# Who turns the output: TensorE or VectorE, in a fused convolution, gated layer and squared layer

## The chip, the core and the metric

The kernel runs on one core of a Trainium2 chip. The metric is the device time of one execution in microseconds (us), as the median of the runs shown. Times in the trace are counted from the first instruction of the profiled execution.

## What is computed

Softmax-weighted causal convolution over 7 tokens (8 heads of 24 channels, 4 batches of 4096 tokens, 192 channels), then a gated layer (192 to 1536 to 192) and a squared-ReLU layer (192 to 2048 to 192), all in fp32:

```python
x_unf = x_pad[:, idx, :].reshape(B, S, K, H, group)
x = np.einsum('hk,bskhg->bshg', softmax(weight), x_unf).reshape(B * S, D)
x = (1 / (1 + np.exp(-(x @ w_gate)))) * (x @ w_val) @ w_out1
h = np.maximum(x @ w_in2, 0.0)
return (h * h) @ w_out2
```

## The kernel before

The 4096 tokens of a batch are cut into 32 blocks of 128; a block holds those 128 tokens of all four batches, so each tile of the hidden layers is 128 features by 512 columns. Channels lie on the partitions throughout. Input tokens are turned into that layout by VectorE in squares of 32 (`transpose_x`, L805: 32 instructions for one block, 16 of 32x128 elements and 16 of 32x64), and the output is turned back at the end.

Each fp32 value is held as a high part (`hi`, a cast by ScalarE) and a low part (`lo`, a subtraction by VectorE), and three products of the parts are summed. Because 192 channels are 128 plus 64, TensorE works in pairs of matmuls, one on the lower 64 partitions and one on the upper 64, that run side by side.

A block goes through two stages. The **gated** stage has T1 = 12 steps. In step t TensorE computes `in1(t)`, 9 pairs (L400, L401) into one of two pairs of PSUM banks of `hp`; ScalarE takes the sigmoid of one bank (L625); VectorE multiplies it by the other bank (`hidden`, L767), which signals `prod_done`; ScalarE casts the product to `hi` (`round_hi`, L611) and VectorE subtracts to get `lo` (`rest_lo`, L781), which signals `lo1_done`. TensorE runs `out1(t - 3)`, 5 pairs (L466 to L472), after `in1(t)`, and after the last step it runs `out1(8)` and `out1(9)` in a row. The **squared** stage has 16 tiles, two per `in2(p)`: ReLU by ScalarE (L628), the square by VectorE (L771), then `hi` and `lo` as above, and `out2` two pairs of tiles behind.

`in1(t)` may begin when the product of tile t - 2 has been read out of its banks (`prod_done`, L435). `out1(t)` begins when `lo` of tile t is there (L486). On VectorE the product of tile t stands ahead of the `lo` of tile t - 1.

The steady loop runs 29 times. One pass is `squared(i - 1)` and then `gated(i + 1)`, so in a gated stage the finished output z of block i - 1 waits to be evacuated, turned and stored:

- step 2: ScalarE copies half of the accumulator (`z_copy`) and VectorE adds (`z_add`, L860) into `z` and `z_parts`;
- SyncE (SP) moves the two halves of `z_parts` that belong to the other partitions (`cross_z`, L290, L291), GpSimd (POOL) adds them (`add_z_rest`, L375), which signals `z_rest_done`;
- TensorE turns the output (`turn`, L493 to L517) after step TR1 = 5: six pairs of transposes into the free banks of `hp`. To have a free pair there, `pair1` flips the parity of the banks from step 6 on;
- ScalarE copies the four pieces to `o_sb` (`turn_copy`, L678, L683), SP stores them (`store`, L295).

Beside that, VectorE in the same gated stage turns the input of the next block (steps 0 to 7, four squares in each), runs its first four convolution taps (EARLY = 4, steps 8 to 11; L812 is the first tap, L815 the others, two instructions each), and at step 8 makes the low part of the second layer's input (`x1_low`, L798). At step 8 ScalarE casts that input (`x1_round`, L659, L661), and GpSimd then computes its remaining low part (`low_of_x1_rest`, L368). The other three taps run in the squared stage (steps 1, 3, 6). SP's order in one pass of the loop is `load_x`, `cross_y1`, `spread_x0`, `cross_z`, `store`, `spread_x1`; `spread_x1` brings the second layer's input to the other partitions and `in2(0)` waits for it.

Outside the loop there are a first gated stage, a second without any output to turn, one light squared and one light gated stage at the end (nothing left to load), and the last squared stage, in which the output of block 30 is turned. The last block's output is turned after all other work.

Of the kernel before, what the change touches and what calls it, by code (L numbers as in the profile page):

```python
# [11 lines left out]
P = 128  # L12
R = 64
# [5 lines left out]
TR1, TR2 = 5, 3  # L19


def conv_gated_squared_mlp(nc, x, weight, w_gate, w_val, w_out1, w_in2, w_out2, out):
# [14 lines left out]
    EARLY = 4  # L37
# [6 lines left out]
    with ExitStack() as ctx:  # L44
# [63 lines left out]


# [31 lines left out]
        sig_w_done = sem("sig_w_done")  # L141
        w_hi = sem("w_hi")
# [16 lines left out]
        sq_done = sem("sq_done")  # L159
# [5 lines left out]
        z_added = sem("z_added")  # L165

# [53 lines left out]

        def pair1(t, prev):

            return (t + (1 if prev and prev[0] == 2 and t > TR1 else 0)) % 2

        def pair2(p, prev):
            return (p + (1 if prev[0] == 2 and p > TR2 else 0)) % 2
# [13 lines left out]
        def _(sp):  # L240
# [47 lines left out]
            def cross_z(j):  # L288
                sp.wait_ge(z_added, 2 * j + (1 if isinstance(j, int) and j == NB - 1 else 2))
                sp.dma_start(z_moved[lower, :, :], z_blocks[upper, :, 0, :]).then_inc(z_crossed, 16)  # L290
                sp.dma_start(z_moved[upper, :, :], z_blocks[lower, :, 1, :]).then_inc(z_crossed, 16)  # L291
# [28 lines left out]
            cross_z(NB - 3)  # L320
            store(NB - 3)
            spread_x1(NB - 2)
# [9 lines left out]
        def _(pool):  # L332
# [38 lines left out]
            def add_z_rest(j):  # L371
                pool.wait_ge(z_crossed, 32 * (j + 1))
                for half, of in enumerate((lower, upper)):
                    v = z_blocks[of, :, half, :]
                    nc.gpsimd.tensor_tensor(v, v, z_moved[of, :, :], ALU.add) \  # L375
                        .then_inc(z_rest_done, 1)
# [17 lines left out]
        def _(pe):  # L394
# [28 lines left out]
            def in1(j, t, prev):  # L423
                turns = prev and prev[0] == 2
# [3 lines left out]
                if t < 2 and turns:  # L428
                    pe.wait_ge(relu_done, T2 * prev[1] + T2 - 2 + 2 * t)
                elif turns and t == TR1 + 1:  # L430
                    pe.wait_ge(prod_done, T1 * j + t)
                elif turns and t == TR1 + 2:
                    pe.wait_ge(turn_copied, 4 * prev[1] + 4)
# [4 lines left out]
                low, up = into(pair1(t, prev), w1, x0_home(j), columns(t))  # L438
                low.then_inc(gate_ready, 1)
                up.then_inc(val_ready, 1)  # L440

            def in2(j, p, prev):
                if p == 0:
                    pe.wait_ge(x1_spread, 48 * j + 48)
                turns = prev[0] == 2
                if p < 2 and not turns:
                    if p == 0:
                        pe.wait_ge(prod_done, T1 * prev[1] + T1)
                elif turns and p == TR2 + 1:
                    pe.wait_ge(relu_done, T2 * j + 2 * p)  # L450
                elif turns and p == TR2 + 2:
                    pe.wait_ge(turn_copied, 4 * prev[1] + 4)
                else:
                    pe.wait_ge(relu_done, T2 * j + 2 * p - 2)
                low, up = into(pair2(p, prev), w2, x1_home(j), columns(p))
                low.then_inc(hid_ready, 1)
                up.then_inc(hid_ready, 1)
# [35 lines left out]
            def turn(j, free):  # L493


                last = isinstance(j, int) and j == NB - 1
                a, b = hp[:, 0, :], hp[:, 1, :]
                pe.wait_ge(*free)
                if last:
                    pe.wait_ge(z_added, 2 * j + 2)  # L500
                else:
                    pe.wait_ge(z_rest_done, 2 * j + 2)
# [5 lines left out]
                if last:  # L508
                    mm.then_inc(turned, 1)
                    a, b = hp[:, 2, :], hp[:, 3, :]  # L510
                    pe.wait_ge(z_rest_done, 2 * j + 2)
                    pe.sem_inc(turn_begun, 1)
# [4 lines left out]
                mm.then_inc(turned, 1 if last else 2)  # L517
# [23 lines left out]
            def gated(j, prev):  # L541
                rest_ = trailing(prev)
                for t in range(T1):
                    if prev is None and t < 2:
                        if t == 0:
                            first_tiles()
                    else:
                        in1(j, t, prev)
                    some_of(rest_)
                    if t >= LAG1:  # L550
                        out1(j, t - LAG1, prev)
                    if prev and prev[0] == 2 and t == TR1:
                        turn(prev[1], (prod_done, T1 * j + t))
                out1(j, T1 - LAG1, prev)

            def squared(j, prev):
# [3 lines left out]
                for p in range(T2P):  # L560
# [5 lines left out]
                    if prev[0] == 2 and p == TR2:  # L566
                        turn(prev[1], (relu_done, T2 * j + 2 * p))
# [21 lines left out]
            turn(NB - 1, (relu_done, T2 * NB))  # L589

        @block.scalar
        def _(act):
# [14 lines left out]
            def round_hi(kind, j, t, prev):  # L607
# [4 lines left out]
                else:  # L612
                    act.wait_ge(sq_done, T2 * j + t + 1)
                    act.copy(hi[:, t % RING, :], hid_t[:, t % 4, :]).then_inc(hi2_done, 1)  # L614

            def activate(kind, j, t, prev):
                if t >= 2 or (prev and prev[0] == kind):
                    s, n = (prod_done, T1) if kind == 1 else (sq_done, T2)
                    act.wait_ge(s, n * j + t - 1)
                elif prev:  # L620
                    s, n = (prod_done, T1) if prev[0] == 1 else (sq_done, T2)
                    act.wait_ge(s, n * prev[1] + n - 1 + t)
                if kind == 1:
                    act.wait_ge(gate_ready, T1 * j + t + 1)
                    act.activation(act_t[:, t % 2, :], hp[:, 2 * pair1(t, prev), :], ACT.Sigmoid).then_inc(sig_done, 1)  # L625
                else:
                    act.wait_ge(hid_ready, T2 * j + t + 1)
                    act.activation(act_t[:, t % 2, :], hp[:, 2 * pair2(t // 2, prev) + t % 2, :], ACT.Relu) \  # L628
# [44 lines left out]
            def turn_copy(j):  # L673
                last = isinstance(j, int) and j == NB - 1
                act.wait_ge(o_room, 16 * (j + 1))
                act.wait_ge(turned, 2 * j + (1 if last else 2))
# [3 lines left out]
                if last:  # L680
                    act.wait_ge(turned, 2 * j + 2)
                for half in range(2):
                    act.copy(o_sb[:, half:B:2, P:D], hp[:, (2 if last else 0) + half, B * R:G * R].rearrange(  # L683
# [12 lines left out]
            def gated(j, prev, pieces_at={}):  # L696
                for t in range(T1):
# [4 lines left out]
                    if t == TR1 + 1 and prev and prev[0] == 2:  # L702
                        turn_copy(prev[1])
# [11 lines left out]
            def squared(j, prev, load_next=True):  # L715
                for t in range(T2):
# [4 lines left out]
                    if t == 2 * TR2 + 2 and prev[0] == 2:  # L721
                        turn_copy(prev[1])
# [5 lines left out]
                    activate(2, j, t, prev)  # L728
                    if t:
# [26 lines left out]
        def _(dve):  # L756
            def hidden(kind, j, t, prev):
# [6 lines left out]
                if kind == 1:  # L764
                    dve.wait_ge(sig_done, T1 * j + t + 1)
                    dve.wait_ge(val_ready, T1 * j + t + 1)
                    dve.tensor_tensor(hid_t[:, t % 4, :], hp[:, 2 * pair1(t, prev) + 1, :], act_t[:, t % 2, :],  # L767
                                      ALU.mult).then_inc(prod_done, 1)
                else:
                    dve.wait_ge(relu_done, T2 * j + t + 1)  # L770
                    dve.tensor_tensor(hid_t[:, t % 4, :], act_t[:, t % 2, :], act_t[:, t % 2, :],  # L771
                                      ALU.mult).then_inc(sq_done, 1)
# [70 lines left out]
            def y1_add(j):  # L843
# [3 lines left out]
                if not (isinstance(j, int) and j < 2):  # L847
                    dve.wait_ge(z_rest_done, 2 * j - 2)
                dve.tensor_tensor(y1_parts[:], acc[:, 1, :], acc_up[:, 1, :], ALU.add).then_inc(y1_added, 1)

            def z_add(j):
                last = isinstance(j, int) and j == NB - 1
                if not (isinstance(j, int) and j == 0):
                    dve.wait_ge(turned, 2 * j)
# [7 lines left out]
            def add_last_z_rest():  # L862
                dve.wait_ge(z_crossed, 32 * NB)
# [4 lines left out]
            def last_of(prev):  # L868
                rest_lo(prev[0], prev[1], (T1 if prev[0] == 1 else T2) - 1)

# [6 lines left out]
            def gated(j, prev, load_next=True):  # L877
                for t in range(T1):
# [24 lines left out]
            def squared(j, prev, load_next=True):  # L903
                for t in range(T2):
# [4 lines left out]
                    if load_next and t in (1, 3, 6):  # L909
                        conv_tap(j + 2, EARLY + t // 2 - t // 6)  # L910
                    if load_next and t == 6:
# [7 lines left out]
                    hidden(2, j, t, prev)  # L919
# [62 lines left out]
```

## Time and profile before

| what | value |
|---|---|
| median of 3 runs | 2385.01 us (2384.59 to 2385.89) |
| profiled execution, its own time | 2385.3 us |
| profiled execution, its span | 2383.1 us |
| TensorE matmul busy | 2351.4 us, 99% |
| TensorE weight load busy | 2119.0 us, 89% |
| VectorE busy | 1824.3 us, 77% |
| ScalarE busy | 1162.3 us, 49% |
| GpSimd busy | 181.9 us, 8% |
| granted TensorE clock | 0.998 of full speed |

The busy time of an instruction in the trace runs from its start to its end; instructions of one engine overlap at their ends, so a duration is longer than the distance to the next start. Where an engine is full, it is the distance between starts that counts. Idle time of an engine is listed with what it waited for. A share over the whole span says nothing of a single stage: VectorE's 77% is a mean over gated and squared stages.

### The profile page before, as it was taken

What the parts mean: (1) busy time and instruction counts of PE and PEld (TensorE: products, weight loads), DVE (VectorE), ACT (ScalarE), POOL (GpSimd) and SP (SyncE); (2) the same over time, 40 slices, a digit from 0 to 9 for tenths busy, and PEclk for the clock granted to TensorE, in tenths of its full rate; (3) what the DMA queues carried; (4) which work ended last, traced back from release to release, by engine and by line L of the source; (5) the groups of instructions that cost most, each with busy time, mean ns of one, the idle gap of its engine ahead of it and who ended that gap; (6) DMA issues with size and microseconds to landing.
All of it is one profiled execution on the core that took longest, in us unless ns stands there. A gap on an engine that the chain in (4) does not pass through costs nothing.

```text
span 2383.1 us, 54234 instructions
## 1 busy us (share of the span) xinstructions
PE 2351.4 (99%) x20880; PEld 2119.0 (89%) x20880; DVE 1824.3 (77%) x3468; ACT 1162.3 (49%) x2208; POOL 181.9 (8%) x164
## 2 busy tenths in 40 slices
PE   6999999999999999999999999999999999999998
PEld 5898998889899989998998888899989888998987
DVE  6777787777787877877777878778777787787755
ACT  3545454454544454544455444455445454454544
POOL 3300000000010000000000000001000000000110
PEclk9999999999999999999999999999999999999999
DMA  5211111111111111111111111111111111111110
GB/s 133 61 48 29 40 48 31 46 29 42 46 38 39 43 28 46 48 31 46 29 42 46 31 46 32 38 46 48 31 46 29 40 48 31 46 29 42 41 39 19
DMA packets 99901, 99.39 MB, mean 42 GB/s; under 512 B 8736, under 2 KB 86048, under 8 KB 99872
## 3 DMA queue, kind: packets, MB, share of 16 engines
q1 hardware_dynamic: 99856, 98.99, 16.9%
q8 instruction: 20, 0.33, 0.1%
q14 instruction: 9, 0.07, 0.0%
q10 hardware_dynamic: 16, 0.00, 0.0%
HBM read 19.27 MB, written 12.58 MB: 13 GB/s over the span
## 4 chain that ended last, share of the span: by engine, by line
PE 98%; DVE 1%; ACT 0%; issue 0%; DMA 0%; POOL 0%; SPq 0%; ACTq 0%; DVEq 0%
PE hp L400 36%; PE hp L401 18%; PE acc L466 17%; PE acc L471 11%; PE acc L467 9%; PE acc L472 6%; DVE y L815 1%; DMA stage<-in_moe_w_val_dram 0%; PE hp L506 0%; PE hp L507 0%; PE hp L515 0%; DVE hid_t L767 0%; POOL wo L358 0%; DMA moved<-z_parts 0%; SPq L263 0%
## 5 line engine op out<-in xcount | busy, mean ns | idle before, releaser
L400 PE MATMUL hp<-xs,w 64*128 64x512 f32 x5760 | 1407.1, 388 | 13.3 <-DVE hid_t L767 5.5
L401 PE MATMUL hp<-xs,w 64*128 64x512 f32 x5760 | 1406.9, 388 | 0.0
L400 PEld LDWEIGHTS hp<-xs,w 64*128 64x128 f32 x5760 | 1060.0, 185 | 121.5 <-DVE hid_t L767 7.4
L401 PEld LDWEIGHTS hp<-xs,w 64*128 64x128 f32 x5760 | 1060.0, 185 | 23.6
L781 DVE TENSOR_TENSOR lo<-hid_t,hi 128x512 fp32r<-128x512 f32 x896 | 617.1, 689 | 7.8
L625 ACT ACTIVATE act_t<-hp 128x512 f32<-128x512 f32 x384 | 230.0, 599 | 674.0 <-PE hp L400 674.0
L771 DVE TENSOR_TENSOR hid_t<-act_t 128x512 f32<-128x512 f32 x512 | 381.6, 746 | 228.4 <-ACT act_t L628 228.1
L466 PE MATMUL acc<-hi,wo 64*128 64x512 f32 x1792 | 549.5, 386 | 0.0
L467 PE MATMUL acc<-hi,wo 64*128 64x512 f32 x1792 | 549.4, 386 | 0.0
L767 DVE TENSOR_TENSOR hid_t<-hp,act_t 128x512 f32<-128x512 f32 x384 | 265.1, 690 | 246.1 <-ACT act_t L625 237.8
L628 ACT ACTIVATE act_t<-hp 128x512 f32<-128x512 f32 x512 | 302.7, 598 | 297.4 <-PE hp L401 180.0
L614 ACT CAST hi<-hid_t 128x512 fp32r<-128x512 f32 x512 | 316.5, 618 | 148.2 <-DVE hid_t L771 142.0
L466 PEld LDWEIGHTS acc<-hi,wo 64*128 64x128 f32 x1792 | 330.0, 184 | 31.4
L472 PE MATMUL acc<-lo,wo 64*128 64x512 f32 x896 | 346.1, 386 | 0.0
L471 PE MATMUL acc<-lo,wo 64*128 64x512 f32 x896 | 346.1, 386 | 0.0
L466 PE MATMUL acc<-lo,wo 64*128 64x512 f32 x896 | 346.1, 386 | 0.0
L467 PE MATMUL acc<-lo,wo 64*128 64x512 f32 x896 | 346.1, 386 | 0.0
L471 PE MATMUL acc<-hi,wo 64*128 64x512 f32 x896 | 346.1, 386 | 0.0
L472 PE MATMUL acc<-hi,wo 64*128 64x512 f32 x896 | 346.1, 386 | 0.0
L467 PEld LDWEIGHTS acc<-hi,wo 64*128 64x128 f32 x1792 | 330.0, 184 | 7.4
L805 DVE STREAM_TRANSPOSE xT<-xin 32x128 f32<-32x128 f32 x960 | 258.0, 269 | 28.2
L611 ACT CAST hi<-hid_t 128x512 fp32r<-128x512 f32 x384 | 235.4, 613 | 11.3 <-DVE hid_t L767 11.3
(69 smaller groups left out, 1897.8 us busy)
## 6 DMA issues: line engine op xcount, KB each, us to landing
xs<-xs SPq DMA_DIRECT2D x160, 256.0 KB, 3.8
xs<-y_rest SPq DMA_DIRECT2D x128, 128.0 KB, 3.1
out_dram<-stage SPq DMA_DIRECT2D x32, 384.0 KB, 2.6
xin<-in_x_dram SPq DMA_DIRECT2D x30, 384.0 KB, 4.2
moved<-y_parts SPq DMA_DIRECT2D x32, 128.0 KB, 2.2
moved<-z_parts SPq DMA_DIRECT2D x64, 64.0 KB, 2.0
stage<-in_moe_w_out_dram SPq DMA_DIRECT2D x7, 384.0 KB, 5.0
stage<-in_moe_w_in_dram SPq DMA_DIRECT2D x12, 128.0 KB, 3.0
```

Of the source, the lines that this page charges most:

```text
L400: low = pe.matmul(hp[:, 2 * pair, :], w[lower, wk, c], xs[lower, xk, :], start=s, stop=e)
L401: up = pe.matmul(hp[:, 2 * pair + 1, :], w[upper, wk, c], xs[upper, xk, :], start=s, stop=e)
L466: pe.matmul(acc[:, 0, :], w[lower], v[lower], start=s, stop=e)
L467: pe.matmul(acc[:, 2, :], w[upper], v[upper], start=s, stop=e)
L471: pe.matmul(acc[:, 1, :], rest_w[lower], v[lower], start=s, stop=e)
L472: mm = pe.matmul(acc[:, 3, :], rest_w[upper], v[upper], start=s, stop=e)
L614: act.copy(hi[:, t % RING, :], hid_t[:, t % 4, :]).then_inc(hi2_done, 1)
L628: act.activation(act_t[:, t % 2, :], hp[:, 2 * pair2(t // 2, prev) + t % 2, :], ACT.Relu) \
L767: dve.tensor_tensor(hid_t[:, t % 4, :], hp[:, 2 * pair1(t, prev) + 1, :], act_t[:, t % 2, :], ALU.mult).then_inc(prod_done, 1)
L771: dve.tensor_tensor(hid_t[:, t % 4, :], act_t[:, t % 2, :], act_t[:, t % 2, :], ALU.mult).then_inc(sq_done, 1)
L781: dve.tensor_tensor(lo[:, t % RING, :], hid_t[:, t % 4, :], hi[:, t % RING, :].bitcast(F32), ALU.subtract).then_inc(done, 1)
L805: dve.transpose(dst, src).then_inc(xT_ready, 1)
```

## The change

1. The turn of the output leaves TensorE for all blocks but the last. VectorE turns it (`turn_z`) in 24 squares of 32x128 straight from `z` and `z_parts` to `o_sb`, three per step in steps 4 to 11 of a gated stage (two per step in steps 4 to 15 of the last squared stage). The flip of banks in `pair1` and `pair2` and the waits around the turn are gone, and so are ScalarE's four copies.
2. In the squared stage ScalarE squares the odd tiles (`square_odd`), VectorE only the even ones.
3. EARLY is 3 instead of 4: the input's squares are spread over steps 0 to 8 and the first tap stands at step 9; four taps fall in the squared stage (steps 1, 3, 5, 7).
4. SP's order in the loop is `cross_z`, `spread_x1`, `store` instead of `cross_z`, `store`, `spread_x1`. The store waits for the 24 squares.
5. `cross_z` moves the upper half of `z_parts` to the lower in one transfer, and GpSimd adds it in one 64x512 instruction instead of two of 64x256.
6. `in2(0)` waits for the product of tile 10 instead of tile 11, since the banks no longer flip.

```diff
-    EARLY = 4
+    EARLY = 3
...
+        for c in range(D // Q):
+            of, ch = (z, slice(c * Q, (c + 1) * Q)) if c < P // Q else (z_parts, slice(c * Q - P, (c + 1) * Q - P))
+            for m in range(P // Q):
+                tok = slice(m * Q, (m + 1) * Q)
+                o_squares.append((of[ch, :].rearrange("c (b s) -> c b s", b=B)[:, :, tok],
+                                  o_sb[tok, :, c * Q:(c + 1) * Q]))
...
             def store(j):
-                sp.wait_ge(turn_copied, 4 * j + 4)
+                if isinstance(j, int) and j == NB - 1:
+                    sp.wait_ge(turn_copied, 4)
+                else:
+                    sp.wait_ge(o_turned, O_SQUARES * (j + 1))
...
                 cross_z(i - 1)
+                spread_x1(i)
                 store(i - 1)
-                spread_x1(i)
...
-                if p < 2 and not turns:
-                    if p == 0:
-                        pe.wait_ge(prod_done, T1 * prev[1] + T1)
...
+                if p < 2 and prev[0] == 1:
+                    pe.wait_ge(prod_done, T1 * prev[1] + T1 - 1 + p)
...
-                    if prev and prev[0] == 2 and t == TR1:
-                        turn(prev[1], (prod_done, T1 * j + t))
...
+            def square_odd(j, t, prev):
...
+                act.wait_ge(relu_done, T2 * j + t + 1)
+                act.activation(hid_t[:, t % 4, :], act_t[:, t % 2, :], ACT.Square).then_inc(odd_sq_done, 1)
...
+            def turn_z(j, part, parts):
+                if part == 0:
+                    dve.wait_ge(o_room, 16 * (j + 1))
+                    dve.wait_ge(z_added, 2 * j + 1)
+                for n in range(part * O_SQUARES // parts, (part + 1) * O_SQUARES // parts):
+                    if n == REST_SQUARES:
+                        dve.wait_ge(z_rest_done, j + 1)
+                    src, dst = o_squares[n]
+                    dve.transpose(dst, src).then_inc(o_turned, 1)
...
+                    if t >= 4 and prev and prev[0] == 2:
+                        turn_z(prev[1], t - 4, T1 - 4)
...
-                    hidden(2, j, t, prev)
+                    if t >= 4 and prev[0] == 2:
+                        turn_z(prev[1], t - 4, T2 - 4)
+                    if t % 2 == 0:
+                        hidden(2, j, t, prev)
```

VectorE's program, from the end of step 6 to the product of step 8 of a gated stage in the loop, before (`xT<-xin` turns the input, `hid_t` is the product, `lo` the low part, `xs<-y,xs` is `x1_low`):

```order
L781 TENSOR_TENSOR lo<-hid_t,hi 128x512
L805 STREAM_TRANSPOSE xT<-xin 32x2x32 x4
L765 REGISTER_ALU
L767 TENSOR_TENSOR hid_t<-hp,act_t 128x512
L781 TENSOR_TENSOR lo<-hid_t,hi 128x512
L834 REGISTER_ALU
L835 REGISTER_ALU
L812 TENSOR_SCALAR y<-xT,taps 128x512
L812 TENSOR_SCALAR y<-xT,taps 128x256
L798 TENSOR_TENSOR xs<-y,xs 128x512
L765 REGISTER_ALU
L767 TENSOR_TENSOR hid_t<-hp,act_t 128x512
```

The same stretch after (`stage<-z` turns the output; `o_sb` lies in the tile `stage`):

```order
L785 TENSOR_TENSOR lo<-hid_t,hi 128x512
L809 STREAM_TRANSPOSE xT<-xin 32x4x32 x4
L883 STREAM_TRANSPOSE stage<-z 32x4x32 x3
L769 REGISTER_ALU
L771 TENSOR_TENSOR hid_t<-hp,act_t 128x512
L785 TENSOR_TENSOR lo<-hid_t,hi 128x512
L809 STREAM_TRANSPOSE xT<-xin 32x2x32 x4
L883 STREAM_TRANSPOSE stage<-z 32x4x32 x3
L802 TENSOR_TENSOR xs<-y,xs 128x512
L769 REGISTER_ALU
L771 TENSOR_TENSOR hid_t<-hp,act_t 128x512
```

Ahead of each product there now stand seven transposes where there were four, the input's last squares have moved into step 8, and the first tap (L812) has moved to step 9.

VectorE in steps 10 and 11 of the same stage, before:

```order
L815 SCALAR_TENSOR_TENSOR y<-xT,taps,y 128x512
L814 REGISTER_ALU
L815 SCALAR_TENSOR_TENSOR y<-xT,taps,y 128x256
L765 REGISTER_ALU
L767 TENSOR_TENSOR hid_t<-hp,act_t 128x512
L781 TENSOR_TENSOR lo<-hid_t,hi 128x512
```

and after:

```order
L819 SCALAR_TENSOR_TENSOR y<-xT,taps,y 128x512
L818 REGISTER_ALU
L819 SCALAR_TENSOR_TENSOR y<-xT,taps,y 128x256
L883 STREAM_TRANSPOSE stage<-z_parts 32x4x32 x3
L769 REGISTER_ALU
L771 TENSOR_TENSOR hid_t<-hp,act_t 128x512
L785 TENSOR_TENSOR lo<-hid_t,hi 128x512
```

Three transposes of the output now stand between each tap and the product.

SP's program in the loop, from `cross_z` on, before:

```order
L290 DMA moved<-z_parts 64x2x128
L291 DMA moved<-z_parts 64x2x128
L294 ISA
L295 ISA
L295 DMA out_dram<-stage 128x4x192
L283 DMA xs<-xs 64x1024
L284 DMA xs<-xs 64x1024
L286 DMA xs<-xs 64x1024
```

and after:

```order
L299 DMA moved<-z_parts 64x512
L287 DMA xs<-xs 64x1024
L288 DMA xs<-xs 64x1024
L290 DMA xs<-xs 64x1024
L305 REGISTER_ALU
L306 ISA
L306 DMA out_dram<-stage 128x4x192
```

The three transfers that feed `in2(0)` now stand ahead of the store.

## Rows read from the trace of the kernel before

**Rows 1.** The page: span, busy time, and the chain that ended last.

```profile
span 2383.1 us, 54234 instructions
PE 2351.4 (99%) x20880; PEld 2119.0 (89%) x20880; DVE 1824.3 (77%) x3468; ACT 1162.3 (49%) x2208; POOL 181.9 (8%) x164
...
PE 98%; DVE 1%; ACT 0%; issue 0%; DMA 0%; POOL 0%; SPq 0%; ACTq 0%; DVEq 0%
```

**Rows 2.** TensorE in order of time around a turn: start us, us, what.

```profile
303.98 0.39 PE L400 MATMUL hp<-xs,w 64*128 64x512 f32 x1
...
307.15 0.21 PE L506 MATMUL hp<-ident,z 64*128 64x64 f32 x1
...
307.59 0.49 PE L400 MATMUL hp<-xs,w 64*128 64x512 f32 x1
...
310.88 0.39 PE L401 MATMUL hp<-xs,w 64*128 64x512 f32 x1
...
314.05 0.39 PE L401 MATMUL hp<-xs,w 64*128 64x512 f32 x1
```

**Rows 3.** TensorE in order of time, where it had waited for a product.

```profile
38.76 0.50 PE L400 MATMUL hp<-xs,w 64*128 64x512 f32 x1 [2.59 <-DVE hid_t L767]
...
39.10 0.39 PE L400 MATMUL hp<-xs,w 64*128 64x512 f32 x1
```

**Rows 4.** VectorE in order of time in a gated stage.

```profile
297.75 1.30 DVE L805 STREAM_TRANSPOSE xT<-xin 32x128 f32<-32x128 f32 x4
299.09 0.69 DVE L767 TENSOR_TENSOR hid_t<-hp,act_t 128x512 f32<-128x512 f32 x1
299.69 0.68 DVE L781 TENSOR_TENSOR lo<-hid_t,hi 128x512 fp32r<-128x512 f32 x1
300.41 1.03 DVE L805 STREAM_TRANSPOSE xT<-xin 32x64 f32<-32x64 f32 x4
...
314.99 1.82 DVE L812 TENSOR_SCALAR y<-xT,taps 128x512 f32<-128x512 f32 x2
316.73 0.68 DVE L798 TENSOR_TENSOR xs<-y,xs 128x512 fp32r<-128x512 f32 x1
...
318.53 1.14 DVE L815 SCALAR_TENSOR_TENSOR y<-xT,taps,y 128x512 f32<-128x512 f32 x2
```

**Rows 5.** All of VectorE's input squares, by shape: count, busy us, mean ns.

```profile
L805 DVE STREAM_TRANSPOSE xT<-xin 32x128 f32<-32x128 f32 x480 | 145.1, 302 | 14.1
L805 DVE STREAM_TRANSPOSE xT<-xin 32x64 f32<-32x64 f32 x480 | 112.9, 235 | 14.1
```

**Rows 6.** ScalarE in order of time: sigmoid of step 7, first ReLUs of the next stage.

```profile
313.15 0.60 ACT L625 ACTIVATE act_t<-hp 128x512 f32<-128x512 f32 x1 [2.07 <-PE hp L400]
...
330.15 1.09 ACT L628 ACTIVATE act_t<-hp 128x512 f32<-128x512 f32 x2 [2.33 <-PE hp L400]
```

**Rows 7.** GpSimd in order of time, same pass of the loop, and one near the end.

```profile
300.48 1.54 POOL L375 TENSOR_TENSOR z_parts<-z_parts,moved 64x256 f32<-64x256 f32 x2 [35.02 <-DMA moved<-z_parts]
315.37 1.28 POOL L368 TENSOR_TENSOR xs<-y_parts,xs 64x512 fp32r<-64x512 f32 x1 [13.35 <-ACT xs L661]
...
2310.85 1.68 POOL L362 TENSOR_TENSOR y_parts<-y_parts,moved 64x512 f32<-64x512 f32 x1 [19.66 <-DMA moved<-y_parts]
```

**Rows 8.** VectorE in order of time: first tap undisturbed, a product TensorE waited for, a `lo` beside GpSimd.

```profile
23.11 0.75 DVE L812 TENSOR_SCALAR y<-xT,taps 128x512 f32<-128x512 f32 x2 [0.99 <-ACT xT L637]
...
38.03 0.68 DVE L767 TENSOR_TENSOR hid_t<-hp,act_t 128x512 f32<-128x512 f32 x1
...
2311.29 1.79 DVE L781 TENSOR_TENSOR lo<-hid_t,hi 128x512 fp32r<-128x512 f32 x1
```

**Rows 9.** SP in order of time: the last of the three transfers of `spread_x1`.

```profile
318.62 0.61 SPq L286 DMA_DIRECT2D xs<-xs  x1
```

**Rows 10.** The page, costliest groups: squares and ReLUs of the squared stage.

```profile
L771 DVE TENSOR_TENSOR hid_t<-act_t 128x512 f32<-128x512 f32 x512 | 381.6, 746 | 228.4 <-ACT act_t L628 228.1
...
L628 ACT ACTIVATE act_t<-hp 128x512 f32<-128x512 f32 x512 | 302.7, 598 | 297.4 <-PE hp L401 180.0
```

More of the change, by code:

```diff
@@ L219, in column_of @@
             return q // 2 + T2P * (q % 2)
[L221 to L226, printed above, removed]
         def x0_home(j):
@@ L371, in add_z_rest @@
             def add_z_rest(j):
[L372 to L376, printed above, removed]
+                pool.wait_ge(z_crossed, 16 * (j + 1))
+                nc.gpsimd.tensor_tensor(z_parts[lower, :], z_parts[lower, :], moved[lower, :], ALU.add) \
+                    .then_inc(z_rest_done, 1)
             for n in range(len(pieces)):
@@ L423, in in1 @@
             def in1(j, t, prev):
-                turns = prev and prev[0] == 2
                 if t == 0:
@@ L427, in in1 @@
                     pe.wait_ge(x0_spread, 64 * j + 64)
-                if t < 2 and turns:
+                if t < 2 and prev and prev[0] == 2:
                     pe.wait_ge(relu_done, T2 * prev[1] + T2 - 2 + 2 * t)
[L430 to L433, printed above, removed]
                 else:
@@ L437, in in1 @@
                     pe.wait_ge(w_lo, split_upto[SECOND_HALF])
-                low, up = into(pair1(t, prev), w1, x0_home(j), columns(t))
+                low, up = into((t % 2), w1, x0_home(j), columns(t))
                 low.then_inc(gate_ready, 1)
@@ L444, in in2 @@
                     pe.wait_ge(x1_spread, 48 * j + 48)
-                turns = prev[0] == 2
-                if p < 2 and not turns:
-                    if p == 0:
-                        pe.wait_ge(prod_done, T1 * prev[1] + T1)
[L449 to L452, printed above, removed]
+                if p < 2 and prev[0] == 1:
+                    pe.wait_ge(prod_done, T1 * prev[1] + T1 - 1 + p)
                 else:
                     pe.wait_ge(relu_done, T2 * j + 2 * p - 2)
-                low, up = into(pair2(p, prev), w2, x1_home(j), columns(p))
+                low, up = into(p % 2, w2, x1_home(j), columns(p))
                 low.then_inc(hid_ready, 1)
@@ L491, in out2, with turn_last @@
                 outward(wo2, column_of(t), t % RING, t == 0, t == T2 - 1, *room(prev)).then_inc(out2_done, 1)
-            def turn(j, free):
-                last = isinstance(j, int) and j == NB - 1
+            def turn_last(j):
                 a, b = hp[:, 0, :], hp[:, 1, :]
[L498 to L502, printed above, removed]
+                pe.wait_ge(relu_done, T2 * NB)
+                pe.wait_ge(z_added, 2 * j + 2)
                 pe.sem_inc(turn_begun, 1)
@@ L507, in turn @@
                     mm = pe.transpose(b[:, to], z[upper, columns(n)], ident[upper, upper])
[L508 to L512, printed above, removed]
+                mm.then_inc(turned, 1)
+                a, b = hp[:, 2, :], hp[:, 3, :]
+                pe.wait_ge(z_rest_done, j + 2)
+                pe.sem_inc(turn_begun, 1)
                 for g in range(B // 2):
@@ L516, in turn @@
                     mm = pe.transpose(b[:, to], z_blocks[upper, g, 1, :], ident[upper, upper])
-                mm.then_inc(turned, 1 if last else 2)
+                mm.then_inc(turned, 1)
             def turn_x(j):
@@ L588, in _ @@
             some_of(rest_)
-            turn(NB - 1, (relu_done, T2 * NB))
+            turn_last(NB - 1)
         @block.scalar
@@ L673, in turn_copy @@
             def turn_copy(j):
-                last = isinstance(j, int) and j == NB - 1
                 act.wait_ge(o_room, 16 * (j + 1))
-                act.wait_ge(turned, 2 * j + (1 if last else 2))
+                act.wait_ge(turned, 1)
                 for half in range(2):
@@ L679, in turn_copy @@
                              hp[:, half, 0:B * R].rearrange("p (b d) -> p b d", b=B)).then_inc(turn_copied, 1)
-                if last:
-                    act.wait_ge(turned, 2 * j + 2)
+                act.wait_ge(turned, 2)
                 for half in range(2):
-                    act.copy(o_sb[:, half:B:2, P:D], hp[:, (2 if last else 0) + half, B * R:G * R].rearrange(
+                    act.copy(o_sb[:, half:B:2, P:D], hp[:, 2 + half, B * R:G * R].rearrange(
                         "p (g d) -> p g d", d=R)).then_inc(turn_copied, 1)
@@ L908, in squared @@
                         evacuate(prev)
-                    if load_next and t in (1, 3, 6):
-                        conv_tap(j + 2, EARLY + t // 2 - t // 6)
-                    if load_next and t == 6:
+                    if load_next and t in (1, 3, 5, 7):
+                        conv_tap(j + 2, EARLY + t // 2)
+                    if load_next and t == 7:
                         keep_halo(j + 2)
```

65 lines of the change are left out of this document (41 added, 24 removed).

## The prediction

> **What bounds the kernel now.** The page comes first: TensorE is busy for 2351.4 of 2383.1 us, and the chain that ended last is 98% TensorE [rows 1]. So only two things can move the time: fewer TensorE columns, or TensorE waiting. The second view is TensorE in order of time. Step 5 of a gated stage starts at 303.98, step 6's first matmul at 307.59, step 7 at 310.88, step 8 at 314.05 [rows 2]. A plain step is 14 pairs in 3.17 us, 0.2268 us a pair. The two steps around the turn take 310.88 - 303.98 = 6.90, and 6.90 - 2 x 3.17 = 0.56 us is what the turn costs: 0.44 for its six pairs (307.15 to 307.59) and the rest to fill the array again. Third, VectorE in order of time, because the change hands it work: its full stretch from 297.75 on shows real distances between starts [rows 4]. Its 77% is a mean and hides that a gated stage is much fuller than a squared one.
>
> **TensorE's part.** 31 turns go, 31 x 0.56 = 17.2 us, all on the path. If nothing waits for longer, the kernel takes 2385.3 - 17.2 = 2368.1 in the profiled execution, 2367.8 by the median (the profiled execution is 0.3 above it, and 2.2 above its own span).
>
> **VectorE's part.** From [rows 4]: product to `lo` 0.60; `lo` to a transpose 0.72, since a transpose starts only when the subtraction has ended; four squares of 32x128 and the step to the product 1.34, so 0.33 each and 0.02; four of 32x64 last 1.03 and with the step to the next 1.06, so 0.26 to 0.27 each; `x1_low`, a subtraction of the same size, 0.60; a pair of taps 1.14 and then 0.04 to a transpose. The means 302 and 235 ns agree, squares hardly overlap [rows 5]. The 24 output squares aren't in the trace; the nearest row is the input square of the same size, so 24 x 0.33 = 7.9 us more in a gated stage. A square can hardly cost less than the smaller input square, 0.27 (6.5 us), unless it overlaps; I take 0.33 and keep 0.27 to 0.37. The tap that moves out gives back 1.1 us. The squares of the hidden tiles that go to ScalarE (8 x 0.75 us [rows 10]) lie in the squared stage, where VectorE had idled, so they buy nothing here. ScalarE's eight squares at about 0.6 us stand against 297 us of idle in front of its ReLUs [rows 10]: cost nothing.
>
> **The running account.** I write what VectorE does in a gated stage against when TensorE needs it, on the clock of the trace without the turn. TensorE's steps would then start at S7 = 310.32, S8 = 313.50, S9 = 316.67, S10 = 319.85, S11 = 323.02. In step t VectorE has 3 to 4 input squares, from step 4 on 3 output squares, the product, the `lo` of t - 1. Starting from 297.75 [rows 4] and adding the distances above, the products start at 298.7, 301.2, 304.5 (step 4), 308.1, 311.2 and 314.9 (step 7); VectorE has no idle time from 297 on. Each is still in time: the product of t has to end before S(t+2).
>
> Then comes GpSimd. Its last subtraction for the second layer starts 2.22 us after the sigmoid of step 7 and takes 1.28 [rows 6, 7]; without the turn that is 314.81 to 316.10. VectorE's `lo` of step 6 wants to start at 315.47, inside it. The rows show what happens: GpSimd adds from 2310.85 to 2312.53, and the `lo` that starts at 2311.29 takes 1.79 instead of 0.68 and ends 0.55 after GpSimd [rows 4, 7, 8]. The input squares beside GpSimd's 300.48 to 302.02 keep their 1.03 [rows 4, 7]. Before the change the first tap met this same GpSimd instruction (1.82 instead of 0.75 [rows 4, 8]) with TensorE well ahead; the tap now stands at step 9 and costs 0.75. So `lo` of step 6 ends at 316.65 and VectorE goes on from 316.70, 0.5 us later than by its own work.
>
> The Trainium skill ("SBUF — State Buffer", section "Who interferes with whom") states this as an exclusive lock: a VectorE instruction with two SBUF inputs and a GpSimd one that reads SBUF block each other for a whole instruction, whichever started first. The rows just given agree. If only some of such meetings blocked, as no row here suggests, the sum would be that of rival (b).
>
> Step 8: 4 x 0.27 + 3 x 0.33 + 0.02 gives `x1_low` at 318.79, product at 319.39, ready at 320.13 (0.69 long, 0.05 to TensorE, as from 38.03 + 0.68 to 38.76 [rows 3, 8]). `in1(10)` wanted 319.85: **0.28 us late**. A restart after a wait costs 0.11 more, as the first pair then takes 0.34 instead of 0.23 [rows 3]. S11 becomes 323.42. Step 9: tap 0.79, squares 1.01, product 322.40, in time. Step 10: tap 1.18, squares, product 325.80, `lo` of step 9 at 326.41, ready 327.15. `out1(9)` wants to start 14 pairs behind S11, at 323.42 + 2.04 + 1.13 = 326.59: **0.56 late**, plus 0.11. `in2(0)` follows at 328.40. Step 11: `lo` of step 10 ready 330.55, `out1(10)` wants it at 330.44: **0.11 late**, plus 0.11. After that the squared stage gives VectorE room (eight squares fewer, one tap more), and it starts the next gated stage with nothing left over. Sum of waits 0.28 + 0.56 + 0.11 + 3 x 0.11 = 1.28 us for each of the 29 full gated stages; against the turn, 1.28 - 0.56 = +0.72. Total: 29 x 0.72 - 2 x 0.56 (the light gated stage and the last squared one only gain) = **+19.8 us**, 2385.0 + 19.8 = 2404.8 us.
>
> **SP and the queues.** `x1_low` ends at 319.5 instead of 317.4, so the three transfers are issued by about 321.3 (before: 318.62 the last [rows 9]) and land some 4 us later, 325.3; `in2(0)` begins at 328.4 (before 327.9, 2.24 ahead of the ReLU at 330.15 [rows 6]). Enough cover, 3 us. Had the store stayed ahead of them, it would have held them until the last output square at 329: that reordering is needed, and it saves nothing against before. `load_x` now waits behind the store until 330; its tile is first used a squared stage later. One transfer instead of two in `cross_z` brings GpSimd's sum forward; the output squares that need it stand at step 9. `in2(0)` waits for an earlier product; before, TensorE did not wait there, so nothing is gained.
>
> **The rivals.** (a) *VectorE keeps up*, the case on the other side. `lo` of step 6 has to start 0.66 sooner to come ahead of GpSimd (315.47 against 314.81); 12 output squares stand before it, so it decides at 0.275 us a square. Then GpSimd waits instead, `lo` of step 9 comes over 1 us sooner, and TensorE never waits: 2367.8. For it: it is a close race. Products and `lo` are 24 x 0.60, input squares 9.6, output squares 7.9, additions 1.2, `x1_low` 0.6, taps 3.0, the extra 0.11 ahead of squares 12 times: 38.0 us in a stage of 168 pairs or 38.1 us. Against it: a row of the same size says 0.33. (b) *GpSimd does not meet a `lo`*, but squares cost 0.33: everything from step 7 on is 0.51 sooner. `in1(10)` is in time; `out1(9)` waits 0.45, `out1(10)` 0.11, restarts 0.22: 0.78, net +0.22, 29 x 0.22 - 1.1 = +5, 2390; with slightly shorter distances 2380. (c) *Output squares dearer*, up to 0.37 (their source rows are 128 elements apart and the target's 192): 9 of them between the GpSimd meeting and `lo` of step 9 add 0.36, net +1.1 per stage, 2415. (d) *The transfers to `in2(0)` come late*: if they landed over 3 us later than I take, each further us would cost 29 us, 2430 or so; nothing in the rows asks for it. (e) *The turn's time doesn't go*: TensorE would have waited there anyway for something else, and the time stays 2385. [Rows 2] speak against it.
>
> **How the numbers follow.** The main case, +0.4 to +1.1 per stage, 2394 to 2416, gets 0.60; (a) 0.19, with some partly waiting between 2368 and 2380; (b) 0.15, split between within and above; (c) and (d) above 2416 0.05; (e) 0.01. A measurement of this kernel can tell about 0.2%, 4.8 us, from no change. Slower by more: 0.60 + 0.05 + 0.03 = 0.68. Faster by more: 0.20. Same: 0.12. The range leaves out the lower part of (a) and the dear ends: 2375 to 2416.
>
> **What would show it.** In the trace after: no transposes of TensorE in the loop; VectorE near 100% busy in gated stages, its output squares 302 ns each; `lo` of step 6 over 1 us long beside GpSimd; TensorE idle for a product or `lo` at steps 10 and 11, some 1 us per pass, and a loop pass of 73.9 us instead of 73.1 (12 x 14 + 8 x 9 + 16 x 5 = 320 pairs of 0.2268, and 0.56). I am wrong if squares of the output are clearly shorter, if that `lo` is 0.68, or if the pass is 72.6.

## The result: 0.7% slower

| | before | after |
|---|---|---|
| median | 2385.16 us | 2400.95 us (2400.18 to 2402.32) |
| ratio to before | | 1.0068, 95% interval 1.0057 to 1.0078 |
| profiled execution, span | 2383.1 us | 2398.6 us |

The changed kernel takes 15.8 us more, and the interval of the ratio lies clear of 1. The forecast was 2404.8 us, 19.8 more, in a range of 2375 to 2416. The line numbers moved: L805 is L809 now, L767 is L771, L781 is L785, L400 is L409, L466 and L471 are L464 and L469, and the new squares of the output are L883.

The page of the kernel after answers [rows 1]: span, busy time, and the engines of the chain that ended last.

```profile
span 2398.6 us, 54220 instructions
PE 2355.5 (98%) x20508; PEld 1918.3 (80%) x20508; DVE 1895.6 (79%) x3956; ACT 1289.8 (54%) x2340; POOL 169.7 (7%) x133
...
PE 91%; DVE 5%; issue 3%; ACT 0%; DMA 0%; POOL 0%; DVEq 0%; SPq 0%; ACTq 0%
```

TensorE has 372 matmuls fewer (31 turns of 12), and yet VectorE has entered the chain with 5%. The page alone doesn't say where; VectorE is busy for 79% of the span, hardly more than the 77% before.

TensorE in order of time (start, duration) shows the place. This is one pass of the loop in the kernel after, at the three seams where it is not back to back. Ends are modelled, so the start distances count, 0.227 us in a steady run.

```profile
319.36 0.39 PE L469 MATMUL acc<-lo,wo 64*128 64x512 f32 x1
...
319.84 0.50 PE L409 MATMUL hp<-xs,w 64*128 64x512 f32 x1
...
320.18 0.40 PE L409 MATMUL hp<-xs,w 64*128 64x512 f32 x1
```

```profile
326.13 0.39 PE L469 MATMUL acc<-lo,wo 64*128 64x512 f32 x1
...
326.80 0.49 PE L464 MATMUL acc<-hi,wo 64*128 64x512 f32 x1 [0.28 <-DVE lo L785]
...
327.13 0.39 PE L464 MATMUL acc<-hi,wo 64*128 64x512 f32 x1
```

```profile
329.88 0.39 PE L409 MATMUL hp<-xs,w 64*128 64x512 f32 x1
...
330.18 0.50 PE L464 MATMUL acc<-hi,wo 64*128 64x512 f32 x1
```

The first seam is `in1(10)`: it starts 0.48 after the pair in front of it instead of 0.23, 0.25 late, and the next pair follows after 0.34, 0.11 more. The second is `out1(9)`: 0.44 late, and 0.10 more. The third is `out1(10)`: 0.07 late, and 0.11 more. That is 1.1 us per pass, and the pairs behind a restart stay a little wide (13 distances of 0.231 from 320.18 to 323.18, against 0.227), so that a pass loses 1.2 in all. Only the second shows as idle time of TensorE in the page's sense; the other two are hidden in the modelled ends, and one finds them only by the distances between starts. The first matmul of the squared stage, which needs SyncE's transfers, comes at 328.06, 0.23 after the pair in front of it: TensorE doesn't wait there. The next lines answer [rows 4]: VectorE in the same gated stage, steps 7 to 10.

```profile
312.14 1.32 DVE L809 STREAM_TRANSPOSE xT<-xin 32x128 f32<-32x128 f32 x4
313.49 0.97 DVE L883 STREAM_TRANSPOSE stage<-z 32x128 f32<-32x128 f32 x3
314.49 0.69 DVE L771 TENSOR_TENSOR hid_t<-hp,act_t 128x512 f32<-128x512 f32 x1
315.10 1.27 DVE L785 TENSOR_TENSOR lo<-hid_t,hi 128x512 fp32r<-128x512 f32 x1
316.40 1.05 DVE L809 STREAM_TRANSPOSE xT<-xin 32x64 f32<-32x64 f32 x4
317.48 0.98 DVE L883 STREAM_TRANSPOSE stage<-z 32x128 f32<-32x128 f32 x3
318.49 0.69 DVE L802 TENSOR_TENSOR xs<-y,xs 128x512 fp32r<-128x512 f32 x1
319.10 0.68 DVE L771 TENSOR_TENSOR hid_t<-hp,act_t 128x512 f32<-128x512 f32 x1
...
325.45 0.69 DVE L771 TENSOR_TENSOR hid_t<-hp,act_t 128x512 f32<-128x512 f32 x1
326.06 0.68 DVE L785 TENSOR_TENSOR lo<-hid_t,hi 128x512 fp32r<-128x512 f32 x1
```

There is no gap in them. The product of step 8 ends at 319.78, and `in1(10)` starts at 319.84; the `lo` of step 9 ends at 326.74, and `out1(9)` starts at 326.80. Both of TensorE's late starts follow VectorE's end by 0.06. And the `lo` at 315.10 takes 1.27 instead of 0.68; GpSimd in the same stretch, the answer to [rows 7], says why:

```profile
314.53 1.28 POOL L379 TENSOR_TENSOR xs<-y_parts,xs 64x512 fp32r<-64x512 f32 x1 [13.52 <-ACT xs L669]
```

It ran from 314.53 to 315.81, and the `lo` ended at 316.37, 0.56 after it.

### The profile page after: what moved, and what is told of

Same layout as the page of the kernel before. It is cut to its first block, busy times and chain, and to the rows that moved or that the text cites. A ratio compares the mean times of both kernels' runs of the same rounds, so it can differ in the third digit from the quotient of the medians.

```text
span 2398.6 us, 54220 instructions
## 1 busy us (share of the span) xinstructions
PE 2355.5 (98%) x20508; PEld 1918.3 (80%) x20508; DVE 1895.6 (79%) x3956; ACT 1289.8 (54%) x2340; POOL 169.7 (7%) x133
## 4 chain that ended last, share of the span: by engine, by line
PE 91%; DVE 5%; issue 3%; ACT 0%; DMA 0%; POOL 0%; DVEq 0%; SPq 0%; ACTq 0%
PE hp L409 51%; PE acc L464 23%; PE acc L469 15%; DVE y L819 2%; DVE lo L785 2%; DVE hid_t L771 1%; PE hp L410 1%; DVE stage L883 0%; PE acc L465 0%; PE acc L470 0%; DMA stage<-in_moe_w_val_dram 0%; DMA moved<-z_parts 0%; POOL wo L369 0%; DVEq L770 0%; SPq L267 0%
## 5 line engine op out<-in xcount | busy, mean ns | idle before, releaser
L409 PE MATMUL hp<-xs,w 64*128 64x512 f32 x5760 | 1406.5, 388 | 16.5 <-DVE hid_t L771 5.7
L409 PEld LDWEIGHTS hp<-xs,w 64*128 64x128 f32 x5760 | 1060.0, 185 | 257.6 <-DVE hid_t L771 21.4
L785 DVE TENSOR_TENSOR lo<-hid_t,hi 128x512 fp32r<-128x512 f32 x896 | 630.8, 707 | 122.0 <-ACT hi L603 118.9
L464 PE MATMUL acc<-hi,wo 64*128 64x512 f32 x1792 | 555.9, 390 | 8.8 <-DVE lo L785 8.8
L464 PEld LDWEIGHTS acc<-hi,wo 64*128 64x128 f32 x1792 | 325.5, 184 | 96.9 <-DVE lo L785 30.7
L771 DVE TENSOR_TENSOR hid_t<-hp,act_t 128x512 f32<-128x512 f32 x384 | 265.1, 690 | 113.4 <-ACT act_t L633 99.4
L464 PE MATMUL acc<-lo,wo 64*128 64x512 f32 x896 | 346.2, 386 | 0.0
L469 PE MATMUL acc<-hi,wo 64*128 64x512 f32 x896 | 346.1, 386 | 0.0
L469 PE MATMUL acc<-lo,wo 64*128 64x512 f32 x896 | 346.1, 386 | 0.0
L465 PEld LDWEIGHTS acc<-hi,wo 64*128 64x128 f32 x1792 | 325.5, 184 | 0.0
L603 ACT CAST hi<-hid_t 128x512 fp32r<-128x512 f32 x512 | 308.9, 609 | 6.1 <-DVE hid_t L775 6.1
L775 DVE TENSOR_TENSOR hid_t<-act_t 128x512 f32<-128x512 f32 x256 | 176.1, 688 | 164.7 <-ACT act_t L636 163.7
L600 ACT CAST hi<-hid_t 128x512 fp32r<-128x512 f32 x384 | 236.2, 615 | 108.3 <-DVE hid_t L771 107.2
L809 DVE STREAM_TRANSPOSE xT<-xin 32x128 f32<-32x128 f32 x960 | 258.5, 269 | 29.2
```

The source lines that it names most:

```text
L409: low = pe.matmul(hp[:, 2 * pair, :], w[lower, wk, c], xs[lower, xk, :], start=s, stop=e)
L464: pe.matmul(acc[:, 0, :], w[lower], v[lower], start=s, stop=e)
L465: pe.matmul(acc[:, 2, :], w[upper], v[upper], start=s, stop=e)
L469: pe.matmul(acc[:, 1, :], rest_w[lower], v[lower], start=s, stop=e)
L771: dve.tensor_tensor(hid_t[:, t % 4, :], hp[:, 2 * (t % 2) + 1, :], act_t[:, t % 2, :], ALU.mult).then_inc(prod_done, 1)
L785: dve.tensor_tensor(lo[:, t % RING, :], hid_t[:, t % 4, :], hi[:, t % RING, :].bitcast(F32), ALU.subtract).then_inc(done, 1)
```

## The experiments

The account of the forecast was theory 1: VectorE is full in the gated stage, and its `lo` of step 6 is locked out by GpSimd. Theory 2 leaves the lock without effect, theory 3 puts the time on ScalarE or SyncE. Pass lengths below are the distance between the same input square in two passes; a pass is 73.13 us in the kernel before (308.16 to 381.29) and 73.74 in the kernel after (312.14 to 385.88).

### GpSimd's instruction made short

```diff
-                low_of_x1_rest(i)
+                low_of_x1_rest(i, 32)
```

The second argument is the number of columns that the subtraction covers.

> The changed kernel, but inside the loop GpSimd's last subtraction for the second layer's input covers 32 of its 512 columns (the rest of that low part is left stale, so this part of the computation is left out). Everything else is as in the changed kernel. Theory 1 (VectorE full in the gated stage, and its low part of step 6 locked out by this GpSimd instruction): the low part of step 6 falls from 1.27 to 0.68 us, all of VectorE behind it moves 0.59 us earlier, TensorE no longer waits at step 10 (0.25 + 0.11 before), and at the two waits that are left it waits about 0.2 + 0.11 and 0.1 + 0.11; a pass falls from 73.73 to about 73.1 us and the time from 2401 to about 2383. Theory 2 (the meeting with GpSimd is harmless, VectorE is simply too full): the same pass and 2401 within 3 us. Theory 3 (ScalarE or SyncE hold TensorE up): 2401 as well.

Measured: 2385.79 us, ratio to before 1.0002 (0.9993 to 1.0012), a pass of 73.19 us. VectorE and GpSimd around the same point in this run:

```profile
316.10 0.68 DVE L785 TENSOR_TENSOR lo<-hid_t,hi 128x512 fp32r<-128x512 f32 x1
316.81 1.05 DVE L809 STREAM_TRANSPOSE xT<-xin 32x64 f32<-32x64 f32 x4
```

```profile
315.53 0.25 POOL L379 TENSOR_TENSOR xs<-y_parts,xs 64x32 fp32r<-64x32 f32 x1 [13.52 <-ACT xs L669]
```

The `lo` is back at 0.68, the wait at step 10 is gone, and two are left (`out1(9)` 0.27 late and `out1(10)` 0.05, each with a restart of 0.11). The meeting with GpSimd costs 0.55 us a pass, 15 us in all: nearly the whole difference between after and before. Theory 2 falls. A pass without any wait takes 72.54 us (the next run); what is left of the waits, 73.19 - 72.54 = 0.65 us a pass, eats the gain of the turn, 0.59. VectorE's fullness alone would have made the change worth nothing.

### Two thirds of the output squares left out

```diff
-                    dve.transpose(dst, src).then_inc(o_turned, 1)
+                    if isinstance(j, int):
+                        dve.transpose(dst, src).then_inc(o_turned, 1)
+                    elif n % 3 == 2:
+                        dve.transpose(dst, src).then_inc(o_turned, 3)
```

> The changed kernel, but inside the loop only one of three output squares is turned, one per step in steps 4 to 11 (two thirds of the output stay unwritten or stale). Theory 1: VectorE has 5.3 us less in a gated stage, the low part of step 6 comes ahead of GpSimd, and TensorE never waits; what is left is the turn that TensorE no longer makes: 31 x 0.56 = 17.2 us less than before the change, 2368. Theory 3: 2401 unless the waits depend on the count of squares.

Measured: 2366.62 us, ratio to before 0.9920 (0.9903 to 0.9936), a pass of 72.54 us (311.12 to 383.66). None of the waits is left. The turn was worth what the trace of before said: 73.13 - 72.54 = 0.59 a pass where 0.56 had been worked out.

### All squares back on VectorE

```diff
-                    if t % 2:
-                        square_odd(j, t, prev)
...
-                    if t % 2 == 0:
-                        hidden(2, j, t, prev)
+                    hidden(2, j, t, prev)
```

> The changed kernel with all squares of the second layer back on VectorE (what ScalarE took over is undone). Theory 1: VectorE's gated stage is untouched, and the squared stage has room for 8 more instructions of 0.60 us in its second half; 2401 within 3 us, at most a few us more if VectorE still carries work over into the next gated stage. Theory 3 (ScalarE's extra squares delay the casts, and so the low parts that TensorE waits for): the time falls, towards 2385 or below.

Measured: 2403.21 us, ratio to before 1.0074 (1.0057 to 1.0091). TensorE's three seams in the gated stage are the same (`in1(10)` 0.24 late, `out1(9)` 0.49, `out1(10)` 0.07). ScalarE's share of the squares neither causes the waits nor relieves them while the output squares stand in the gated stage.

### The kernel before with odd squares on ScalarE

```diff
                     activate(2, j, t, prev)
+                    if t % 2:
+                        square_odd(j, t, prev)
...
-                    hidden(2, j, t, prev)
+                    if t % 2 == 0:
+                        hidden(2, j, t, prev)
```

> The kernel before with one part of the change alone: ScalarE squares the odd tiles of the second layer. Theory 1: VectorE only idles more in the squared stage, and TensorE didn't wait there: 2385 within 2 us. Theory 3 (ScalarE's squares cost TensorE time): over 2390.

Measured: 2385.67 us, ratio 1.0001 (0.9991 to 1.0010). This part of the change alone is worth nothing, and costs nothing. With the run before, the ScalarE half of theory 3 falls. The SyncE half falls with the runs above, in which SyncE's order is that of the changed kernel and the waits shrink or go when GpSimd or VectorE has less to do.

### Four early taps

```diff
-    EARLY = 3
+    EARLY = 4
...
-                    if load_next and t in (1, 3, 5, 7):
-                        conv_tap(j + 2, EARLY + t // 2)
+                    if load_next and t in (1, 3, 6):
+                        conv_tap(j + 2, EARLY + t // 2 - t // 6)
...
-                    if load_next and t == 7:
+                    if load_next and t == 6:
```

> The changed kernel with EARLY back at 4: the input squares stand in steps 0 to 7, the first tap at step 8, one more pair of taps in the gated stage. Theory 1: VectorE has 1.1 us more in the gated stage; the low part of step 6 now wants to start at about 316.2, behind GpSimd's end at 315.8, so it isn't locked out (0.59 less), but four input squares more stand ahead of it; the product of step 8 comes about as late as now, and the low part of step 9 about 0.5 us later: some 0.5 us more a pass, 2410 to 2418. If only the meeting with GpSimd mattered: 2385.

Measured: 2407.59 us, ratio 1.0093 (1.0077 to 1.0110), a pass of 73.94 us. The direction held, but the size was less than half of what was expected, 0.2 us a pass instead of 0.5, and the time is below the range of 2410 to 2418. The `lo` of step 6 came too late to meet GpSimd:

```profile
317.15 0.68 DVE L785 TENSOR_TENSOR lo<-hid_t,hi 128x512 fp32r<-128x512 f32 x1
317.75 0.74 DVE L816 TENSOR_SCALAR y<-xT,taps 128x512 f32<-128x512 f32 x2
```

GpSimd's instruction ran from 315.76 to 317.04, beside squares and a product from PSUM, and nothing was held up. TensorE has four seams now: `in1(10)` and `in1(11)` 0.05 late, `out1(9)` 0.65, `out1(10)` 0.03, and 0.11 more at each. The waits add up to 0.78 us against 0.76 in the changed kernel, and there is one restart more. So the meeting isn't needed for the slowdown: with one more pair of taps in the gated stage VectorE's work alone costs as much. That part of the change, one tap less in the gated stage, had saved 6.6 us.

### SyncE's old order

```diff
-                spread_x1(i)
-                store(i - 1)
+                store(i - 1)
+                spread_x1(i)
```

> The changed kernel with SyncE's old order in the loop (store ahead of the second layer's spread). Theory 1: the spread is issued only after the last output square, about 9.8 us later than now (329.0 instead of 319.2), its three transfers then land at about 335 and the second layer's first matmul, due at 328.1, waits some 6 to 7 us in each of 29 passes: 2401 + 29 x 6.5 = about 2590, with SyncE named behind TensorE's wait. If the order did not matter: 2401.

Measured, in a single execution: 2691.07 us. TensorE at the first matmul of the squared stage, with what it waited for:

```profile
359.89 0.79 PE L409 MATMUL hp<-xs,w 64*128 64x512 f32 x1 [7.46 <-DMA xs<-xs]
...
360.48 0.62 PE L409 MATMUL hp<-xs,w 64*128 64x512 f32 x1
...
360.91 0.62 PE L409 MATMUL hp<-xs,w 64*128 64x512 f32 x1
```

The order does what the forecast said: SyncE must have the spread ahead of a store that waits for step 11. The cost was underestimated, 10.0 us a pass (290.5 us of span over 29) where 6.5 had been expected. The wait was 7.5 us instead of 6.5, and after it the pairs were 0.43 us apart instead of 0.23: the granted clock had fallen. Busy time, clock and DMA share by stretch, in that run:

```profile
300.00:355.00 55.00, 52.05 (x455) 43.31 (x452) 43.04 (x99) 24.61 (x44) 2.57 (x2) 1.00 0.07 16
355.00:360.00 5.00, 0.10 (x2) 0.11 (x2) 0.12 (x1) 0.00 (x0) 0.00 (x0) 0.70 0.96 242
360.00:365.00 5.00, 5.00 (x28) 4.01 (x30) 0.30 (x1) 0.93 (x2) 0.00 (x0) 0.62 0.07 24
365.00:370.00 5.00, 5.00 (x46) 4.49 (x44) 4.29 (x8) 3.97 (x8) 0.00 (x0) 1.00 0.11 24
```

The column behind GpSimd's is the clock: 1.00, then 0.70 and 0.62 around and behind the idle stretch, then 1.00 again. A distance of 0.43 is that of the lower of the two levels, 1.2 GHz instead of 2.4. Nine distances at it or near it (0.59 the first, 0.40 the last) make 1.9 us. With a first matmul 7.6 us late by its start, that is 9.5 of the 10.0; some later passes stayed at 0.43 for longer, as the one from 2115.47, with fifteen such distances.

### The output turned one stage later

If VectorE is full in one stage and idle in another, the squares belong in the other. Here z of block i - 2 is turned in steps 8 to 15 of the squared stage of the next pass, three squares a step, and stored there.

```diff
-                    if t >= 4 and prev and prev[0] == 2:
-                        turn_z(prev[1], t - 4, T1 - 4)
...
+                    if t >= 8 and turned_block is not None:
+                        turn_z(turned_block, t - 8, T2 - 8)
...
-                squared(i - 1, (1, i))
+                squared(i - 1, (1, i), turned_block=i - 2)
...
                 spread_x0(i + 1)
+                store(i - 2)
                 cross_z(i - 1)
                 spread_x1(i)
-                store(i - 1)
```

> The changed kernel, but VectorE turns the output of a block one stage later: three squares in each of the steps 8 to 15 of the next squared stage, and SyncE stores it there (the loop's first pass stands ahead of the loop). Nothing is left out. Theory 1: the gated stage has 7.9 us less and no wait of TensorE for a product or a low part; the squared stage has room, since VectorE idles 7.8 us in its second half and 3.3 us at the start of the gated stage; 31 x 0.56 = 17.2 us less than before the change, 2368, and 33 us less than the changed kernel. If VectorE's squares cost TensorE time in any stage (by their number, not by their place), it stays near 2400.

Measured: 2367.23 us, ratio to before 0.9919 (0.9903 to 0.9936). This beats both kernels, by 18 us and by 34 us, and is where a kernel without any turn on TensorE ends (2366.6 with most squares left out). VectorE in the second half of the squared stage:

```profile
349.62 0.97 DVE L889 STREAM_TRANSPOSE stage<-z 32x128 f32<-32x128 f32 x3
350.62 0.69 DVE L791 TENSOR_TENSOR lo<-hid_t,hi 128x512 fp32r<-128x512 f32 x1
351.35 0.97 DVE L889 STREAM_TRANSPOSE stage<-z 32x128 f32<-32x128 f32 x3
352.35 0.69 DVE L781 TENSOR_TENSOR hid_t<-act_t 128x512 f32<-128x512 f32 x1
352.96 0.68 DVE L791 TENSOR_TENSOR lo<-hid_t,hi 128x512 fp32r<-128x512 f32 x1
```

The same number of squares, the same 0.33 us each, and TensorE doesn't notice. What cost time was that many squares in that place: a third of them in the gated stage cost nothing (2366.62), and all of them in the squared stage cost nothing either.

This run also has a meeting with GpSimd in the gated stage. It falls on `x1_low`, another subtraction with two SBUF inputs:

```profile
317.61 1.03 DVE L808 TENSOR_TENSOR xs<-y,xs 128x512 fp32r<-128x512 f32 x1
```

```profile
316.81 1.28 POOL L385 TENSOR_TENSOR xs<-y_parts,xs 64x512 fp32r<-64x512 f32 x1 [13.47 <-ACT xs L675]
```

It takes 1.03 instead of 0.69 and ends 0.55 after GpSimd, as the `lo` did in the changed kernel, and TensorE has no wait. In these runs the meeting cost time only where VectorE was full already.

### The same, with all squares of the hidden tiles on VectorE

The edit is that of the run with all squares back on VectorE, made on the kernel above.

> As the run with the turn in the squared stage, and VectorE makes all squares of the hidden tiles too. Theory 1: VectorE then has about 8 x 0.60 = 4.8 us more in the squared stage, some 38 us of work against TensorE's 34.5; 3 us go over into the gated stage, which idles 3.3 us at its start, so TensorE begins to wait a little at the change of stages: 2370 to 2390. It tells what ScalarE's share is worth once the output squares stand there. If it is worth nothing: 2368.

Measured: 2395.91 us, ratio 1.0039 (1.0025 to 1.0054). It is slower than expected; I had allowed 2370 to 2390. VectorE's surplus is paid before it reaches the gated stage's own tiles; TensorE waits at three seams of a pass, 0.08, 0.21 and 0.21 late with 0.10 to 0.11 more at each, all of them in `out2`, the last one behind `in1(0)` of the gated stage. The second, at 360.89 instead of 360.68, comes 0.05 after the end of a `lo` of the squared stage (360.16 + 0.68):

```profile
360.45 0.39 PE L475 MATMUL acc<-lo,wo 64*128 64x512 f32 x1
...
360.89 0.50 PE L470 MATMUL acc<-hi,wo 64*128 64x512 f32 x1
```

ScalarE's odd squares, worth nothing in the kernel before, are worth 29 us in this one. They are what makes room for the output squares in the squared stage; the changed kernel made the room there and then put the squares in the other stage.

## Why the prediction was right

**The turn's price** (0.56 a pass, from the distance between two plain steps and two with a turn) measured 0.59, when nothing took its place. The product 31 x 0.56 is 17.4 and not the 17.2 of the forecast; the 0.2 us don't matter.

**The output square at 0.33 us**, taken from the input square of the same size, held: 496 of them take 303 ns and 248 take 302 ns each, and three with the step to the next instruction take 1.00 (317.48 to 318.49, the answer to [rows 5]).

**The running account.** The forecast had the `lo` of step 6 at 315.47, GpSimd at 314.81 and the end of both meetings at 316.65; in the trace after, counted from the same plain start of step 6 (307.15 in the forecast's clock, 306.90 in the trace, 0.25 earlier), they are at 315.35, 314.78 and 316.62. The product of step 8 was forecast for 319.39 and came at 319.35.

**The waits.** Forecast 0.28, 0.56 and 0.11 late, measured 0.25, 0.44 and 0.07; forecast 0.11 for each restart, measured 0.11, 0.10 and 0.11. The waits and restarts come to 1.08 us where 1.28 had been forecast. Both errors at `out1(9)` point the same way: VectorE took 0.06 less from the product of step 8 to the `lo` of step 9 than in the account (6.96 against 7.02), and TensorE 0.06 more from `in1(10)` to the moment at which it wanted `out1(9)` (6.52 against 6.46). The second is a term that the account lacked: after a restart the pairs stay 0.231 us apart for a while. Over a pass such wider distances come to some 0.1 us, so a pass was 1.20 us longer than one without waits (73.74 - 72.54). Against the kernel before, a pass grew by 0.61 us and not by 0.72; over 29 passes that is 3.2 of the 3.9 us between 2404.8 and 2400.95. So the number is a little better than its terms, since waits put too high and a term left out partly cancel. A wait is the small difference of two long sums: 0.06 us, 1% of either sum, is a seventh of the 0.44 here.

**The lock.** The step that carried the sign was GpSimd's instruction; without it the forecast's rival (b) gave 2390, and the run with the short instruction gave 2385.8. The Trainium skill ("SBUF — State Buffer", section "Who interferes with whom") says that a VectorE instruction with two SBUF inputs and a GpSimd one that reads SBUF exclude each other, while one with at most one SBUF input is free, unless it runs in a mode that takes both ports; it counts `tensor_scalar` among those that can. Trace and runs agree: 1.27 us instead of 0.68 for the `lo`, and no delay of squares and PSUM products beside GpSimd in the run with four early taps. The exception fits too: in the kernel before it was a `tensor_scalar`, the first tap, that took 1.82 instead of 0.75. What happens to GpSimd where VectorE started first was not looked at.

**Rival (a), VectorE keeps up,** was to decide at 0.275 us a square. The squares are 0.33, so it didn't come about; with a third of them VectorE keeps up, and the time it gave, 2367.8, is 1.2 from the 2366.6 measured.

**SyncE's queue.** `x1_low` and the three transfers went as forecast or 0.7 us sooner (the last issued at 320.37, which is 320.62 on the forecast's clock, where 321.3 had been written), and nobody waited for them. That the reordering was needed is shown by the run without it. The expectation of that run put its price too low: the wait was 1 us longer, and the lower clock after it was left out.

**Not forecast:** the rivals held no case in which the same squares stand in another stage. That was no part of the change, but the account already had all the numbers for it.

## What to carry to other kernels

Before work goes to an engine that is 77% busy, make the account stage by stage, with the distances between starts of a full stretch and with the moment at which the bounding engine needs each result; the mean hides that one stage is full while VectorE idles for 7.8 of 18 us in the next (the changed kernel from 345 to 363). Put moved work in the stage with room, even one stage later, and free that room where the work will stand. Look also at what GpSimd does at that moment: one of its SBUF instructions meeting one VectorE instruction with two SBUF inputs cost 0.55 us a pass here, nearly the 0.59 that the whole turn saved.

## What the runs showed of the hardware

- A wait of TensorE costs more than its length. Each seam with a wait lost 0.10 to 0.11 us more on the next pair (0.33 to 0.34 instead of 0.23), also where it waited for only 0.07 us.
- A VectorE subtraction of 128x512 with two SBUF inputs that meets GpSimd's SBUF instruction ends 0.55 to 0.56 us after it: the `lo` of the changed kernel, `x1_low` with the turn in the squared stage, and a `lo` of the kernel before (2311.29 + 1.79 against 2310.85 + 1.68).
- After an idle stretch of 7.5 us the granted clock was 0.70 and then 0.62 in stretches of 5 us, and pairs were 0.43 us apart instead of 0.23 until it came back to 1.00. The waits of some tenths of a microsecond in the other runs left the mean granted clock at 0.996 to 0.999, as in the kernel before.
- Square on ScalarE, from SBUF, took its place beside ReLU in the squared stage at no visible cost while VectorE made no output squares there: 2385.67 against 2385.49 for the kernel before in the same series.
